# The two row halves of TensorE run opposite products in step, instead of one half trailing the other

## The chip, the cores and the metric

The program runs on one core of a Trainium2 chip. The metric is the time of the kernel on the device in microseconds (us). One profiled execution is shown beside the timed ones: its span runs from the first to the last event on the core. Engines are TensorE (PE, its weight loads PEld), VectorE (DVE), ScalarE (ACT), GpSimd (POOL) and SyncE (SP), which only starts transfers.

## The reference

The input `x` is 2 x 4096 tokens of 192 channels. A causal convolution over 7 tokens comes first, with one softmaxed set of taps for each of 8 heads (24 channels a head). Two feed-forward layers of width 2048 follow:

```python
x = conv(x, softmax(weight))                 # 8192 tokens x 192
h = x @ w_in;   y = max(0.01 * h, h) @ w_out             # "leaky" layer
h = y @ w_in2                                            # "smooth" layer
g = 0 where h <= -1;  h where h >= 1;  (h + 1)**2 / 4 between
out = g @ w_out2
```

All operands are fp32. The kernel splits each operand into a rounded part (hi) and the rest (lo) and adds the products that matter, so that one product becomes several matmuls.

## The kernel before

**Tiles and jobs.** Tokens are worked in 16 tiles of 512. A tile passes two layers, each one is a job: 32 jobs of 16 chunks, a chunk being 128 of the 2048 hidden columns. Job 0 and 1 are leaky jobs of the tiles 0 and 1; then smooth and leaky jobs alternate; jobs 30 and 31 are smooth.

**A chunk.** The first product fills `hidden[c % 4]` (one PSUM bank of four). ACT copies it to `pre` (L767; in a smooth job a Relu, L769, and a Square, L774), DVE makes `g` (L1079 or L1084), ACT rounds it to `g_hi` (`round_g`, L786), DVE subtracts for `g_lo` (L1090). The second product adds the chunk to `acc_edge` and `acc_main`. Two chunks `c`, `c + 1` are always handled together: DVE makes both `g_lo` after the second `g`.

**TensorE in halves.** A contraction of 128 rows is cut into the rows 0 to 63 (`top`) and 64 to 127 (`bottom`), which run as separate 64-row matmuls side by side and add into the same bank one after the other. For two chunks the first product takes 9 matmuls in each half and the second 10 (4 on `acc_edge`, 6 on `acc_main`). `two_chunks(job, c)` writes 19 pairs of one matmul for each half by hand; I call such a place a slot, and one call of `two_chunks` a round. In a round, slots 0 to 8, the top half makes the first product of `c` and `c + 1`, and in slots 9 to 18 the second product of `c - 4` and `c - 3`. The bottom half follows the top: it adds its part of the first product in slots 8 to 16, and its part of the second product in slots 17 and 18 and, in the next round, 0 to 7. Banks pass from half to half by the semaphores `hidden_top_made`, `edge_top_added`, `edge_bottom_added`, `main_top_added` and `main_bottom_added`.

**What holds ACT.** `g_hi` and `g_lo` have four buffers each. ACT may round chunk `c` only once the second product of chunk `c - 4` is complete: `round_g` waits for `main_bottom_added`.

**Work between.** A smooth job's ACT and DVE streams carry the work of other tiles at fixed chunks: the taps of the next tile's convolution (`edge_tap`, chunks 0 to 6), its rounding (`main_hi`, `edge_hi` at chunk 7, `main_lo`, `edge_lo` at chunk 8: L1002, L1054, L1062), and the turn-over of a leaky result into the next operand (`take_edge`, `round_between` on ACT at chunk 9: L803, L808; `between_sum` at chunk 10, `between_main` and `between_edge_hi` at chunk 11 on DVE: L1096, L1102, L1109). Job 0 and 1 also round 16 pieces of weights (ACT L850 to L857, POOL L423 to L433) that SP loads.

**The ends.** The first chunks of job 0 are written in `opening`. After the last round the bottom half finishes its trailing part alone, and the last four chunks' second product runs on the whole array (`whole_edge`, `whole_main`: L611 to L625).

Of the kernel before, what the change touches and what calls it, by code (L numbers as in the profile page):

```python
# [24 lines left out]
P = 128  # L25
T = 512
# [9 lines left out]
JOB_0_MAIN_TAPS = {0: 1, 1: 2, 2: 3, 3: 4, 4: 5, 5: 6}  # L36
JOB_0_EDGE_TAPS = {7: (0,), 8: (1,), 9: (2, 3), 10: (4,), 11: (5, 6)}
PIECE_AT = ({1: 3, 3: 4, 5: 5, 7: 6, 9: 7, 13: 8}, {1: 9, 3: 10, 7: 11, 9: 12, 11: 13, 13: 14, 15: 15})
TAP_LAST = (1, 3)
# [15 lines left out]
def bass_conv_mlp_mlp(nc, x, weight, moe_w_in, moe_w_out, moe2_w_in, moe2_w_out, out):  # L55
# [24 lines left out]
    with ExitStack() as ctx:  # L80
# [106 lines left out]
        hidden_top_made = sem("hidden_top_made")  # L187
        edge_top_added = sem("edge_top_added")
# [83 lines left out]
        last_main = hidden[3][:, 0:T - SPLIT]  # L272
# [40 lines left out]
        def _(sp):  # L313
# [49 lines left out]
            load_w_out(1)  # L363
            load_x_edge(ODD, 0)
            load_w_out(2)
            for piece in range(AHEAD, 2 * PIECES):
                sp.wait_ge(stage_used, piece - AHEAD + 1)
                load_w_in(piece)
# [21 lines left out]
        def _(pool):  # L390
# [52 lines left out]
            low_w_out(2)  # L443
            low_w_out(AHEAD)
            for n in (0, 1):
                for c, piece in PIECE_AT[n].items():
                    if piece > AHEAD:
                        pool.wait_ge(g_lo_ready, CHUNKS * n + c + 1)
                        low_w_in(piece)
                        low_w_out(piece)  # L450
# [10 lines left out]
        def _(pe):  # L461
# [6 lines left out]
            def top_first(job, c, i):  # L468
# [6 lines left out]
                if is_number(n, 0) and c == 0:  # L475
                    if i == 0:
                        pe.wait_ge(main_rounded, 1)
                        pe.wait_ge(first_rounded, 1)
                        pe.wait_ge(w_in_hi, 1)
                    if i == 1:  # L480
                        pe.wait_ge(first_main_ready, 1)
                    if i == 2:
                        pe.wait_ge(weights_ready, 1)
                    if i == 3:
                        pe.wait_ge(edge_hi_ready, 2)
# [25 lines left out]
            def bottom_first(job, c, i):  # L511
# [4 lines left out]
                if i == 0:  # L516
                    pe.wait_ge(hidden_top_made, CHUNKS * n + c + 1)
# [5 lines left out]
                elif i == 3:  # L523
                    last = c % 2 == 0
                    if is_number(n, 0, 1) and c == 0:
                        pe.wait_ge(op1_ready, n + 1)
# [16 lines left out]
            def top_second(job, c, i):  # L543

# [5 lines left out]
                w, hi, lo = w_out[l][top, k], g_hi[k % SLOTS][top, :], g_lo[k % SLOTS][top, :]  # L550
                edge, main = acc_edge[a], acc_main[a]
                if i == 0:
                    if is_number(n, 0, 2):
                        pe.wait_ge(stage_used, l_piece(n, c) + 1)
                    if c == 0 and reached(n, 2):
                        pe.wait_ge(acc_taken, n - 1)
                    if c > 0:
                        pe.wait_ge(edge_bottom_added, (PAIRS - 1) * n + c // 2)
# [3 lines left out]
                elif i in (1, 3):  # L562
                    pe.wait_ge(g_lo_ready, CHUNKS * n + k + 1)
                    done = nc.tensor.matmul(edge[:], w[:, P:2 * P], lo, start=False, stop=False)  # L564
                    if i == 3:
                        done.then_inc(edge_top_added, 1)
                elif i in (4, 7):
                    if i == 4 and c > 0:
                        pe.wait_ge(main_bottom_added, (PAIRS - 1) * n + c // 2)
# [3 lines left out]
                else:  # L573
                    done = nc.tensor.matmul(main[:], w[:, 0:P], lo, start=False, stop=False)  # L574
                    if i == 9:
                        done.then_inc(main_top_added, 1)

            def bottom_second(job, c, i):
# [6 lines left out]
                w, hi, lo = w_out[l][bottom, k], g_hi[k % SLOTS][bottom, :], g_lo[k % SLOTS][bottom, :]  # L585
                edge, main = acc_edge[a], acc_main[a]
                if i in (0, 2):
                    if i == 0:
                        pe.wait_ge(edge_top_added, PAIRS * n + c // 2 + 1)
                    nc.tensor.matmul(edge[:], w[:, P:2 * P], hi, start=False, stop=False)  # L590
                elif i in (1, 3):
                    done = nc.tensor.matmul(edge[:], w[:, P:2 * P], lo, start=False, stop=last and i == 3)  # L592
                    if i == 3:
                        done.then_inc(acc_edge_ready if last else edge_bottom_added, 1)
                elif i in (4, 7):
                    if i == 4:
                        pe.wait_ge(main_top_added, PAIRS * n + c // 2 + 1)
# [3 lines left out]
                else:  # L601
                    done = nc.tensor.matmul(main[:], w[:, 0:P], lo, start=False, stop=last and i == 9)  # L602
                    if i == 9:
                        done.then_inc(acc_main_ready if last else main_bottom_added, 1)
# [24 lines left out]
            def second_half(job, c):  # L629

                for i in range(3):
                    top_second(job, c - 4, i)
                    bottom_first(job, c, i + 1)
                for i in range(5):
                    top_second(job, c - 4, i + 3)
                    bottom_first(job, c + 1, i)
                for i in range(2):
                    top_second(job, c - 4, i + 8)  # L640
                    bottom_second(job, c - 4, i)

            def opening(job):

                for c, i in ((0, 0), (0, 2), (1, 0), (1, 2), (0, 1), (0, 3), (0, 4)):
                    top_first(job, c, i)
                for i in range(2):
                    top_first(job, 1, 2 * i + 1)  # L650
                    bottom_first(job, 0, i)
                for i in range(2):
                    top_first(job, 2, i)
                    bottom_first(job, 0, i + 2)
                for i in range(3):
                    top_first(job, 2, i + 2)
                    bottom_first(job, 1, i)
                for i in range(2):
                    top_first(job, 3, i)
                    bottom_first(job, 1, i + 3)  # L660
                for i in range(2):
                    top_first(job, 3, i + 2)
                    bottom_first(job, 2, i)
                for i in range(2):
                    top_first(job, 4, i)
                    bottom_first(job, 2, i + 2)
                for i in range(3):
                    top_first(job, 4, i + 2)
                    bottom_first(job, 3, i)
                for i in range(2):  # L670
                    top_first(job, 5, i)
                    bottom_first(job, 3, i + 3)
                for i in range(2):
                    top_first(job, 5, i + 2)
                bottom_first(job, 4, 0)
                second_half(job, 4)

            def two_chunks(job, c):

                for i in range(5):
                    top_first(job, c, i)
                    bottom_second(job, c - 6, i + 2)
                for i in range(3):
                    top_first(job, c + 1, i)
                    bottom_second(job, c - 6, i + 7)
                top_first(job, c + 1, 3)
                bottom_first(job, c, 0)
                second_half(job, c)  # L690

            def run(job):
                opens = is_number(job["n"], 0)
                if opens:
                    opening(job)
                for c in range(6 if opens else 0, CHUNKS, 2):
# [50 lines left out]
        def _(act):  # L747
# [13 lines left out]
            def before(job, c):  # L761
# [3 lines left out]
                act.wait_ge(hidden_ready, k + 1)  # L765
# [486 lines left out]
```

## Time and profile before

| | us |
|---|---|
| median of 3 runs (lowest to highest) | 1123.32 (1122.94 to 1123.82) |
| the profiled execution's own time | 1123.96 |
| its span | 1122.2 |
| PE busy in the span | 1117.6 |
| DVE busy | 897.8 |
| ACT busy | 799.1 |
| POOL busy | 53.8 |

Busy times add what overlaps within an engine's pipeline, so an engine at 80% may have fewer free moments than it seems. A row of a timeline has the start, the duration, the engine, the line and the tiles written and read; `x2` merges instructions that follow at once; the bracket says how long the engine stood still before it and what ended that.

### The profile page before, as it was taken

The numbers are of one execution on the slowest core, as the hardware profiler recorded it, in microseconds if no ns is written. First come the engines' busy times: TensorE is split into PE (matmuls) and PEld (weight loads), VectorE is DVE, ScalarE is ACT, GpSimd is POOL, SyncE is SP. The second block draws the span as 40 slices with busy tenths as digits, with TensorE's granted clock in tenths as the row PEclk, the third lists the DMA queues.
The fourth block names the chain that finished last, engine by engine and source line by source line (L and its number), as shares of the span: only waits on it lengthen the run. The fifth ranks groups of instructions, "written<-read, shape, count | busy, mean of one in ns | idle before, by whom it ended". The sixth has DMA issues, their size and how long they took to land.

```text
span 1122.2 us, 25759 instructions
## 1 busy us (share of the span) xinstructions
PE 1117.6 (100%) x9758; PEld 1102.8 (98%) x9758; DVE 897.8 (80%) x1512; ACT 799.1 (71%) x1476; POOL 53.8 (5%) x86
## 2 busy tenths in 40 slices
PE   9999999999999999999999999999999999999998
PEld 8889999999999999999999999999999999999998
DVE  7888877788778887788878888887788877888665
ACT  6878677586775857768577675866758677686786
POOL 7451000000000000000000000000000000000000
PEclk9999999999999999999999999999999999999999
DMA  6330100101001010010100101010010100100001
GB/s 143 103 76 2 27 4 2 30 2 29 2 1 30 1 30 1 3 28 1 29 1 11 21 1 30 1 15 16 1 30 1 26 6 1 30 1 15 1 1 29
DMA packets 112872, 21.95 MB, mean 20 GB/s; under 512 B 104048, under 2 KB 112752, under 8 KB 112752
## 3 DMA queue, kind: packets, MB, share of 16 engines
q1 hardware_dynamic: 110192, 19.81, 9.6%
q8 instruction: 77, 1.26, 0.5%
q10 hardware_dynamic: 2560, 0.52, 0.2%
q14 instruction: 43, 0.35, 0.1%
HBM read 14.02 MB, written 6.29 MB: 18 GB/s over the span
## 4 chain that ended last, share of the span: by engine, by line
PE 100%; DVE 0%; ACT 0%; issue 0%
PE hidden L506 11%; PE hidden L500 7%; PE hidden L504 7%; PE hidden L502 7%; PE acc_main L570 7%; PE acc_main L574 7%; PE acc_main L572 7%; PE acc_edge L564 7%; PE acc_edge L561 7%; PE acc_main L602 3%; PE acc_main L600 3%; PE acc_main L598 3%; PE hidden L520 3%; PE hidden L522 3%; PE hidden L518 3%; PE hidden L527 3%
## 5 line engine op out<-in xcount | busy, mean ns | idle before, releaser
L786 ACT CAST g_hi<-g 128x512 fp32r<-128x512 f32 x510 | 299.5, 618 | 267.2 <-PE acc_main L602 198.5
L1090 DVE TENSOR_TENSOR g_lo<-g,g_hi 128x512 fp32r<-128x512 f32 x510 | 335.1, 690 | 93.9 <-ACT g_hi L786 89.1
L1084 DVE SCALAR_TENSOR_TENSOR g<-hidden,pre 128x512 f32<-128x512 f32 x256 | 176.7, 690 | 101.5 <-ACT pre L774 96.1
L506 PE MATMUL hidden<-op_edge,w_edge 64*128 64x512 f32 x768 | 255.8, 386 | 0.0
L518 PE MATMUL hidden<-op_hi,w_main 64*128 64x512 f32 x512 | 197.9, 387 | 0.0
L500 PE MATMUL hidden<-op_hi,w_main 64*128 64x512 f32 x512 | 197.9, 386 | 0.0
L522 PE MATMUL hidden<-op_hi,w_main 64*128 64x512 f32 x512 | 197.9, 386 | 0.0
L527 PE MATMUL hidden<-op_edge,w_edge 64*128 64x512 f32 x512 | 197.7, 386 | 0.0
L520 PE MATMUL hidden<-op_lo,w_main 64*128 64x512 f32 x512 | 197.7, 386 | 0.0
L502 PE MATMUL hidden<-op_lo,w_main 64*128 64x512 f32 x512 | 197.7, 386 | 0.0
L504 PE MATMUL hidden<-op_hi,w_main 64*128 64x512 f32 x512 | 197.7, 386 | 0.0
L564 PE MATMUL acc_edge<-g_lo,w_out 64*128 64x512 f32 x508 | 196.2, 386 | 0.0
L598 PE MATMUL acc_main<-g_hi,w_out 64*128 64x512 f32 x508 | 196.2, 386 | 0.0
L590 PE MATMUL acc_edge<-g_hi,w_out 64*128 64x512 f32 x508 | 196.2, 386 | 0.0
L592 PE MATMUL acc_edge<-g_lo,w_out 64*128 64x512 f32 x508 | 196.1, 386 | 0.0
L574 PE MATMUL acc_main<-g_lo,w_out 64*128 64x512 f32 x508 | 196.1, 386 | 0.0
L570 PE MATMUL acc_main<-g_hi,w_out 64*128 64x512 f32 x508 | 196.1, 386 | 0.0
L602 PE MATMUL acc_main<-g_lo,w_out 64*128 64x512 f32 x508 | 196.1, 386 | 0.0
L572 PE MATMUL acc_main<-g_hi,w_out 64*128 64x512 f32 x508 | 196.1, 386 | 0.0
L600 PE MATMUL acc_main<-g_hi,w_out 64*128 64x512 f32 x508 | 196.1, 386 | 0.0
L561 PE MATMUL acc_edge<-g_hi,w_out 64*128 64x512 f32 x508 | 196.1, 386 | 0.0
L1079 DVE SCALAR_TENSOR_TENSOR g<-hidden,pre 128x512 f32<-128x512 f32 x256 | 172.6, 680 | 16.5 <-ACT pre L767 13.3
(143 smaller groups left out, 2784.8 us busy)
## 6 DMA issues: line engine op xcount, KB each, us to landing
x_in<-in_x_dram SPq DMA_DIRECT2D x65, 64.0 KB, 2.2
out_dram<-y_main SPq DMA_DIRECT2D x60, 64.0 KB, 1.8
stage<-in_moe_w_out_dram SPq DMA_DIRECT2D x16, 192.0 KB, 2.9
x_in_edge<-in_x_dram SPq DMA_DIRECT2D x66, 32.0 KB, 1.9
stage<-in_moe_w_in_dram SPq DMA_DIRECT2D x32, 64.0 KB, 2.4
out_dram<-y_edge SPq DMA_DIRECT2D x32, 64.0 KB, 1.8
stage<-in_moe_w_in_dram SPq DMA_DIRECT2D x15, 128.0 KB, 2.4
x_in<-in_x_dram ACTq DMA_DIRECT2D x3, 64.0 KB, 3.3
```

What stands on the lines that cost most here:

```text
L500: nc.tensor.matmul(h[:], w_main[l][top, 0, cols], op_hi[l][b][top, :], start=True, stop=False)
L502: nc.tensor.matmul(h[:], w_main[l][top, 0, cols], op_lo[l][b][top, :], start=False, stop=False)
L504: nc.tensor.matmul(h[:], w_main[l][top, 1, cols], op_hi[l][b][top, :], start=False, stop=False)
L506: done = nc.tensor.matmul(h[:], w_edge[l][top, i - 3, cols], op_edge[l][b][top, :], start=False, stop=False)
L518: nc.tensor.matmul(h[:], w_main[l][bottom, 0, cols], op_hi[l][b][bottom, :], start=False, stop=False)
L561: nc.tensor.matmul(edge[:], w[:, P:2 * P], hi, start=k == 0, stop=False)
L564: done = nc.tensor.matmul(edge[:], w[:, P:2 * P], lo, start=False, stop=False)
L570: nc.tensor.matmul(main[:], w[:, 0:P], hi, start=k == 0, stop=False)
L572: nc.tensor.matmul(main[:], w[:, 2 * P:], hi, start=False, stop=False)
L574: done = nc.tensor.matmul(main[:], w[:, 0:P], lo, start=False, stop=False)
L786: nc.scalar.copy(hi_of(n, c)[:], g[c % SLOTS][:]).then_inc(g_hi_ready, 1)
L1090: nc.vector.tensor_tensor(lo_of(n, c)[:], g[c % SLOTS][:], hi_of(n, c)[:].bitcast(F32), ALU.subtract).then_inc(g_lo_ready, 1)
```

## The change

`two_chunks` keeps its 19 slots, but the halves are set against each other: while the top half makes the first product of `c` and `c + 1` (slots 0 to 8), the bottom half starts the second product of `c - 4` and `c - 3` (slots 0 to 9); then the top half completes that second product (slots 9 to 18), and the bottom half completes the first one (slots 10 to 18). No part is left to the next round.

```diff
             def two_chunks(job, c):
                 for i in range(5):
                     top_first(job, c, i)
-                    bottom_second(job, c - 6, i + 2)
-                for i in range(3):
+                    bottom_second(job, c - 4, i)
+                for i in range(4):
                     top_first(job, c + 1, i)
-                    bottom_second(job, c - 6, i + 7)
-                top_first(job, c + 1, 3)
-                bottom_first(job, c, 0)
-                second_half(job, c)
+                    bottom_second(job, c - 4, i + 5)
+                top_second(job, c - 4, 0)
+                bottom_second(job, c - 4, 9)
+                for i in range(4):
+                    top_second(job, c - 4, i + 1)
+                    bottom_first(job, c, i)
+                for i in range(5):
+                    top_second(job, c - 4, i + 5)
+                    bottom_first(job, c + 1, i)
```

The bottom half now opens the second product, so it is the one that waits for `g_hi_ready`, `g_lo_ready` and `acc_taken`; the top half closes it, and ACT's wait names it:

```diff
             def round_g(n, c):
                 if c % 2 == 0 and not ends(n, c):
                     if c >= 4:
-                        act.wait_ge(main_bottom_added, (PAIRS - 1) * n + c // 2 - 1)
+                        act.wait_ge(main_top_added, (PAIRS - 1) * n + c // 2 - 1)
```

`opening` now holds the first six chunks, written out pair by pair (`both((0, 0), (1, 0))`: the top half works on chunk 0 while the bottom half works on chunk 1, then they swap), with waits for `halves_opened` where they swap. ACT then waits for two halves in either order. In job 0 the convolution of tile 1, its rounding and the weights' pieces stand at later or other chunks, with w_in and w_out rounded apart:

```diff
-JOB_0_MAIN_TAPS = {0: 1, 1: 2, 2: 3, 3: 4, 4: 5, 5: 6}
-JOB_0_EDGE_TAPS = {7: (0,), 8: (1,), 9: (2, 3), 10: (4,), 11: (5, 6)}
+JOB_0_MAIN_TAPS = {3: (1, 2), 5: (3, 4), 7: (5, 6)}
+JOB_0_EDGE_TAPS = {9: (0, 1), 10: (2,), 11: (3, 4), 12: (5, 6)}
...
-                    if is_number(n, 0) and c == 11:
+                    if is_number(n, 0) and c == 13:
                         edge_hi(job["finish"])
                         edge_low(job["finish"])
-                    if is_number(n, 0) and c == 13:
+                    if is_number(n, 0) and c == 14:
                         edge_top(job["finish"])
...
-                        if c == 13:
+                        if c == 14:
                             edge_lo(job["finish"])
```

At the end the eight matmuls of the bottom half alone are gone, and the whole-array part runs pair by pair of chunks:

```diff
-            for i in range(2, 10):
-                bottom_second(last_jobs[-1], CHUNKS - 6, i)
-            for c in range(CHUNKS - 4, CHUNKS):
-                whole_edge(JOBS - 1, 1, SMOOTH, c)
-            for c in range(CHUNKS - 4, CHUNKS):
-                whole_main(JOBS - 1, 1, SMOOTH, c)
+            for pair in (CHUNKS - 4, CHUNKS - 2):
+                for c in (pair, pair + 1):
+                    whole_edge(JOBS - 1, 1, SMOOTH, c)
+                for c in (pair, pair + 1):
+                    whole_main(JOBS - 1, 1, SMOOTH, c)
```

TensorE, before, where a round reaches the second product: from the last first-product matmul of the top half (L506, slot 8) to slot 12.

```order
L506 MATMUL hidden<-op_edge,w_edge 128x512
L518 MATMUL hidden<-op_hi,w_main 128x512 [waits hidden_top_made]
L561 MATMUL acc_edge<-g_hi,w_out 128x512 [waits g_hi_ready,edge_bottom_added]
L520 MATMUL hidden<-op_lo,w_main 128x512
L564 MATMUL acc_edge<-g_lo,w_out 128x512 [waits g_lo_ready]
L522 MATMUL hidden<-op_hi,w_main 128x512
L561 MATMUL acc_edge<-g_hi,w_out 128x512 [waits g_hi_ready]
L527 MATMUL hidden<-op_edge,w_edge 128x512
L564 MATMUL acc_edge<-g_lo,w_out 128x512 [waits g_lo_ready]
```

The waits for `g_hi` and `g_lo` stand at slots 9 to 12 of the round. TensorE, changed, slots 0 to 3 of a round, the first product's matmuls of the top half being L495 to L501 and those of the bottom half on the second product L555 and L558:

```order
L495 MATMUL hidden<-op_hi,w_main 128x512 [waits g_ready]
L555 MATMUL acc_edge<-g_hi,w_out 128x512 [waits g_hi_ready,edge_top_added]
L497 MATMUL hidden<-op_lo,w_main 128x512
L558 MATMUL acc_edge<-g_lo,w_out 128x512 [waits g_lo_ready]
L499 MATMUL hidden<-op_hi,w_main 128x512
L555 MATMUL acc_edge<-g_hi,w_out 128x512 [waits g_hi_ready]
L501 MATMUL hidden<-op_edge,w_edge 128x512
L558 MATMUL acc_edge<-g_lo,w_out 128x512 [waits g_lo_ready]
```

The same four waits now stand at the round's first four slots, nine slots ahead of where they stood. ACT, before, late in job 0: the casts of tile 1 (L829 to L844) and the `pre` of chunks 12 to 15 (L767).

```order
L829 CAST op_edge<-conv_edge 64x256 [waits edge_tapped]
L830 CAST op_edge<-conv_edge 64x256
L837 CAST op_top<-op_edge 64x256 [waits edge_hi_ready]
L767 COPY pre<-hidden 128x512 [waits hidden_ready] x2
L786 CAST g_hi<-g 128x512 [waits main_bottom_added,g_ready]
L786 CAST g_hi<-g 128x512 [waits g_ready]
L850 CAST w_main<-stage 128x256 [waits stage_loaded2]
L851 CAST w_edge<-stage 128x256
L857 CAST w_out<-stage 128x2x192 [waits rows_loaded2]
L844 CAST op_top<-op_edge 64x256 [waits edge_hi_ready]
L767 COPY pre<-hidden 128x512 [waits hidden_ready] x2
```

ACT, changed, the same place (casts L899 to L914, `pre` L837, weights L920 to L927), from chunk 13's `g_hi` to chunk 15's `pre`:

```order
L856 CAST g_hi<-g 128x512 [waits g_ready]
L920 CAST w_main<-stage 128x256 [waits stage_loaded2]
L921 CAST w_edge<-stage 128x256
L927 CAST w_out<-stage 128x2x192 [waits rows_loaded1]
L899 CAST op_edge<-conv_edge 64x256 [waits edge_tapped]
L900 CAST op_edge<-conv_edge 64x256
L907 CAST op_top<-op_edge 64x256 [waits edge_hi_ready]
L837 COPY pre<-hidden 128x512 [waits hidden_ready]
L914 CAST op_top<-op_edge 64x256 [waits edge_hi_ready]
L837 COPY pre<-hidden 128x512 [waits hidden_ready]
```

The three casts moved from ahead of chunk 12's `pre` to between the weights and chunk 14's `pre`, and the fourth between the `pre` of 14 and 15.

## Rows read from the trace of the kernel before

**Rows 1.** The page's first part: busy us, share, count.

```profile
PE 1117.6 (100%) x9758; PEld 1102.8 (98%) x9758; DVE 897.8 (80%) x1512; ACT 799.1 (71%) x1476; POOL 53.8 (5%) x86
```

**Rows 2.** Stretches: PE, PEld, DVE, ACT, POOL busy (count), clock, DMA, GB/s.

```profile
80.00:90.00 10.00, 10.00 (x91) 9.03 (x89) 9.74 (x15) 8.14 (x16) 7.48 (x11) 1.00 0.09 15
100.00:1100.00 1000.00, 1000.00 (x8827) 1000.00 (x8824) 801.12 (x1347) 708.65 (x1286) 0.00 (x0) 1.00 0.08 12
```

**Rows 3.** Waits of ACT: for whom, us in total, times, longest.

```profile
ACT g_hi L786 <- PE acc_main L602: 198.5, 165, 1.7
```

**Rows 4.** Timeline of PE in smooth job 6, one round and more.

```profile
235.32 0.39 PE L527 MATMUL hidden<-op_edge,w_edge 64*128 64x512 f32 x1
...
237.08 0.39 PE L500 MATMUL hidden<-op_hi,w_main 64*128 64x512 f32 x1
...
241.39 0.39 PE L500 MATMUL hidden<-op_hi,w_main 64*128 64x512 f32 x1
...
248.41 0.39 PE L564 MATMUL acc_edge<-g_lo,w_out 64*128 64x512 f32 x1
```

**Rows 5.** Timeline of ACT in smooth job 6, chunks 7 to 10.

```profile
232.74 0.58 ACT L769 ACTIVATE pre<-hidden 128x512 f32<-128x512 f32 x1
...
236.44 0.60 ACT L769 ACTIVATE pre<-hidden 128x512 f32<-128x512 f32 x1
...
240.65 0.62 ACT L786 CAST g_hi<-g 128x512 fp32r<-128x512 f32 x1 [0.88 <-DVE g L1084]
241.30 0.58 ACT L803 COPY edge_b<-acc_edge 64x512 f32<-64x512 f32 x1
```

**Rows 6.** Timeline of DVE in smooth job 6, chunks 6 to 11.

```profile
235.88 1.29 DVE L1090 TENSOR_TENSOR g_lo<-g,g_hi 128x512 fp32r<-128x512 f32 x2
...
239.93 0.69 DVE L1084 SCALAR_TENSOR_TENSOR g<-hidden,pre 128x512 f32<-128x512 f32 x1
...
243.69 0.69 DVE L1084 SCALAR_TENSOR_TENSOR g<-hidden,pre 128x512 f32<-128x512 f32 x1 [1.69 <-ACT pre L774]
...
246.42 1.28 DVE L1090 TENSOR_TENSOR g_lo<-g,g_hi 128x512 fp32r<-128x512 f32 x2
```

**Rows 7.** Timeline of DVE, then PE, where PE once waited for `g_lo`.

```profile
27.24 1.24 DVE L1090 TENSOR_TENSOR g_lo<-g,g_hi 128x512 fp32r<-128x512 f32 x2
...
28.54 0.49 PE L564 MATMUL acc_edge<-g_lo,w_out 64*128 64x512 f32 x1
28.55 0.50 PE L518 MATMUL hidden<-op_hi,w_main 64*128 64x512 f32 x1
28.88 0.39 PE L570 MATMUL acc_main<-g_hi,w_out 64*128 64x512 f32 x1
```

**Rows 8.** Timeline of DVE and PE early in job 2.

```profile
82.98 1.55 DVE L1090 TENSOR_TENSOR g_lo<-g,g_hi 128x512 fp32r<-128x512 f32 x2
...
84.76 0.39 PE L564 MATMUL acc_edge<-g_lo,w_out 64*128 64x512 f32 x1
```

**Rows 9.** Timeline of ACT, then DVE, late in job 0.

```profile
40.74 0.41 ACT L837 CAST op_top<-op_edge 64x256 fp32r<-64x256 f32 x1
...
43.11 0.42 DVE L1054 TENSOR_TENSOR op_edge<-conv_edge,op_edge 64x256 fp32r<-64x256 f32 x1
...
45.84 1.29 DVE L1079 SCALAR_TENSOR_TENSOR g<-hidden,pre 128x512 f32<-128x512 f32 x2 [0.55 <-ACT pre L767]
...
50.31 1.29 DVE L1090 TENSOR_TENSOR g_lo<-g,g_hi 128x512 fp32r<-128x512 f32 x2 [0.18 <-ACT g_hi L786]
```

**Rows 10.** Timeline of PE at its two ends, and DVE's last `g_lo`.

```profile
12.34 0.49 PE L500 MATMUL hidden<-op_hi,w_main 64*128 64x512 f32 x1
...
1110.71 0.39 PE L534 MATMUL hidden<-op_top,w_edge 64*128 64x512 f32 x1
...
1113.23 1.46 DVE L1090 TENSOR_TENSOR op_lo<-g,op_hi 128x512 fp32r<-128x512 f32 x2
...
1117.75 0.39 PE L625 MATMUL acc_main<-op_lo,w_out 128*128 128x512 f32 x1
```

More of the change, by code:

```diff
@@ L363, in _ @@
             load_w_out(1)
+            sp.wait_ge(weights_ready, 1)
+            load_w_in(AHEAD)
             load_x_edge(ODD, 0)
@@ L549, in top_second @@
                 k = c + (i // 2 if i < 4 else (i - 4) // 3)
-                w, hi, lo = w_out[l][top, k], g_hi[k % SLOTS][top, :], g_lo[k % SLOTS][top, :]
+                w, hi, lo = w_out[l][bottom, k], g_hi[k % SLOTS][bottom, :], g_lo[k % SLOTS][bottom, :]
                 edge, main = acc_edge[a], acc_main[a]
@@ L584, in bottom_second @@
                 last = c == CHUNKS - 2
-                w, hi, lo = w_out[l][bottom, k], g_hi[k % SLOTS][bottom, :], g_lo[k % SLOTS][bottom, :]
+                w, hi, lo = w_out[l][top, k], g_hi[k % SLOTS][top, :], g_lo[k % SLOTS][top, :]
                 edge, main = acc_edge[a], acc_main[a]
@@ new lines, in first_part @@
+            def first_part(c, i, part):
+                cols = slice(c * P, (c + 1) * P)
+                if i == 0:
+                    w, x_part = w_main[LEAKY][part, 0, cols], op_hi[LEAKY][EVEN]
+                elif i == 1:
+                    w, x_part = w_main[LEAKY][part, 0, cols], op_lo[LEAKY][EVEN]
+                elif i == 2:
+                    w, x_part = w_main[LEAKY][part, 1, cols], op_hi[LEAKY][EVEN]
+                else:
+                    x_part = op_top[LEAKY][EVEN] if part is bottom and i == 4 else op_edge[LEAKY][EVEN]
+                    w = w_edge[LEAKY][part, i - 3, cols]
+                goes_first = part is (top, bottom)[c % 2]
+                return nc.tensor.matmul(hidden[c % SLOTS][:], w, x_part[part, :], start=goes_first and i == 0,
+                                        stop=not goes_first and i == 3)
@@ new lines, in both, with opened, made, edge_part @@
+            def both(t, b):
+                return first_part(*t, top), first_part(*b, bottom)
+            def opened(halves):
+                halves[0].then_inc(halves_opened, 1)
+                halves[1].then_inc(halves_opened, 1)
+            def made(halves):
+                halves[0].then_inc(hidden_ready, 1)
+                halves[1].then_inc(hidden_ready, 1)
+            def edge_part(k, low, part):
+                g_part = (g_lo if low else g_hi)[k]
+                return nc.tensor.matmul(acc_edge[0][:], w_out[LEAKY][part, k, P:2 * P], g_part[part, :],
+                                        start=part is top and k == 0 and not low, stop=False)
@@ L694, in run @@
                 if opens:
-                    opening(job)
-                for c in range(6 if opens else 0, CHUNKS, 2):
+                    opening()
+                for c in range(OPEN if opens else 0, CHUNKS, 2):
                     two_chunks(job, c)
@@ L1155, in run @@
                     if is_number(n, 0):
-                        if c in JOB_0_MAIN_TAPS and c not in TAP_LAST:
-                            main_tap(job["load"], JOB_0_MAIN_TAPS[c])
-                        if c == 5:
+                        if c == 8:
                             turn_x_edge(job["load"])
```

216 lines of the change are left out of this document (125 added, 91 removed).

## The prediction, made before the changed kernel was run

> **What bounds the kernel now.** I read the page's first part, the stretches, the waits, and then the timelines of PE, ACT and DVE over one smooth job. PE works without a break: in the 1000 us from 100 on it issues 8827 half matmuls and never stands still, at a granted clock of 1.00, which is 2.4 GHz [rows 1, 2]. Two round starts of the same kind lie 4.31 us apart (237.08 and 241.39, with 19 slots between), so one slot is 0.2267 us [rows 4]. Alone in the array, in step or one behind the other, the halves keep this pace, so pairing them otherwise saves no slot inside the loop. The top half does 32 x 16 x 9.5 - 20 = 4844 matmuls, 1098.1 us at this pace, out of a span of 1122.2.
>
> ACT looks idle because it waits for PE: 198.5 us of `g_hi` waits for the release of a buffer [rows 3]. That is spare time on ACT, but not in front of PE. The reader should look for the spare between `g_lo` and the matmul that reads it. In smooth job 6 the `g_lo` of chunks 10 and 11 end at 246.42 + 1.28 = 247.70 [rows 6], and the matmul on chunk 11's starts at 248.41 [rows 4]. A matmul that has to wait costs a little more than the wait: where it happened, `g_lo` ended at 28.48, the matmul started at 28.54, the other half stood as well (28.55), and the next followed 0.34 later instead of 0.23 [rows 7]. So a late `g_lo` delays PE's stream to its own end plus 0.06 + 0.11 = 0.17. The spare of chunk 11 is 248.41 - 247.87 = 0.54 us.
>
> **The change, part by part.**
>
> *The loop.* The waits for `g_hi` and `g_lo` move from slots 9 to 12 to slots 0 to 3 of the same round: nine slots, 2.04 us, less time for ACT and DVE. At the other end the first product is complete at slots 13 and 18 instead of 11 and 16. Whether this costs anything is decided at the longest way from a finished `hidden` to a `g_lo`, which in a smooth job runs from chunk 8 to chunk 11, since on it stand the other tiles' steps: Relu of 8 at 236.44 [rows 5], Square, `g` of 8, three roundings of the next tile, `g` of 9 at 239.93 [rows 6], `g_hi` of 9 at 240.65, L803 and L808 at once behind it [rows 5], Relu and Square of 10, `g` of 10 at 243.69, the sum, `g` of 11, two more steps, and both `g_lo` to 247.70 [rows 6]. Each link follows the one before within some 0.03 us (239.93 + 0.69 = 240.62, then 240.65); no wait for PE stands in it. It takes 247.70 - 236.44 = 11.26 us and cannot shrink, as both engines go from one link to the next.
>
> The changed schedule gives it less. From the start of the matmul that completes chunk 8 (slot 13) to the one that reads `g_lo` of chunk 11 (slot 3, three rounds on) are 57 - 10 = 47 slots, 10.65 us. Needed are the matmul itself 0.39, 0.03 to ACT, 11.26, and 0.17 to PE: 11.85. PE stands for 1.20 us. A check from the other side: spare 0.54, less 2.04, plus 0.25 because the Relu of 8 began later (236.44) than `hidden` would allow it even with slot 13 (235.32 + 0.45 + 0.39 + 0.03 = 236.19 [rows 4]), plus the 0.06 by which the bottom half trails: -1.19. Both halves wait, since a matmul behind the waiting one in PE's queue waits as well [rows 7]. This recurs in the 14 smooth jobs that carry both kinds of steps: 14 x 1.20 = 16.8 us. The nearest rows bound one such stall at 0 (the chain hidden as now) and 1.5 (nothing of the late Relu regained); I take 1.20, with 0.9 to 1.4 for the range. Job 30 lacks the next tile's roundings: 0 to 1.2, taken as 0.2. Job 31 and the leaky jobs have no such chain: 0.
>
> *ACT's release.* `round_g` now waits for the top half's end of the second product, slot 18 of the round, where it was slot 7 of the next. It comes 8 slots earlier, but is not in the chain: nothing, hidden behind the `g` of the same pair.
>
> *Jobs 0 and 1.* Early in job 2 DVE is 9.74 of 10 us busy [rows 2]. There the last `g_lo` of job 1 ends at 84.53, and the matmul on it starts at 84.76 [rows 8]: with 0.17 for the way, the spare is 0.06. DVE dictates this matmul now and will then; but it stands nine slots earlier in its round. So all later rounds start 2.04 - 0.06 = 1.98 us later, plus whatever DVE itself is late. What PE lost or won before, in the opening and through job 0, is swallowed by this. DVE's own delay comes late in job 0: three casts of 0.41 to 0.43 move in front of chunk 14's `pre`, which DVE already waits for, and the two subtractions of 0.43 move from ahead of a pair of `g_lo` to between the `g` of 14 and 15 [rows 9]. That is 1.28 + 0.86 = 2.14 at most and 0 at least; DVE stood idle for 0.55 and 0.18 around there [rows 9], which leaves 1.41. I take 1.3. The same number of DVE, ACT and POOL instructions is issued; SP issues as many transfers, with w_in of a piece now ahead of its w_out, and weights arrive while PE still works on the pieces before. I count both as 0, hidden behind DVE's lateness; uncovered they would add what they are late.
>
> *The end.* Before, the last chunk's first product starts its last matmul at 1110.71, slot 16, and the last matmul of all starts at 1117.75 [rows 10], 7.04 later, eight matmuls of the bottom half alone among it (1.81). After, that matmul is at slot 18, 0.45 later. Then 10 whole matmuls on chunks 12 and 13 follow, but those on 14 and 15 wait for DVE: `g_lo` of 15 ends at 1113.23 + 1.46 = 1114.69 [rows 10], 3.98 behind the matmul; with 0.17, and six more matmuls of 0.23, the last starts 5.51 behind it. Gained: 7.04 - 5.51 - 0.45 = 1.08, call it 1.1; bounds 0 and 1.81.
>
> *Sum.* 1.98 + 1.3 + 16.8 + 0.2 - 1.1 = 19.2 us. The profiled execution took 1123.96 for a span of 1122.2; the median of the runs is 0.64 lower, 1123.32. I predict 1123.3 + 19.2 = 1142.5.
>
> **The rivals.**
>
> *More places stall.* In the same job the pair 6 and 7 comes close: Relu of 7 at 232.74 [rows 5], `g_lo` at 235.88 + 1.29 = 237.17 [rows 6]: 4.43, with 0.39, 0.03 and 0.17 it is 5.02 of 23 slots or 5.21 us. Spare 0.19. If ACT or DVE come to it 0.5 us later, since the stream behind a stall is packed more tightly, it adds 0.3 x 14 = 4, and a second such place as much: 1151. Against it: each stall gives both engines 1.2 us to catch up.
>
> *The loop keeps up, only the start is late.* If the chain is 1.2 us shorter on the chip than I read it, 16.8 and 0.2 fall away: 1125.5. For it speaks that ACT is busy for 71% alone [rows 1]; against it that its idle time does not stand in the chain.
>
> *The whole stream of ACT and DVE closes up, and nothing is slower.* It decides from the point at which the chain takes less than 10.65 - 0.59 = 10.06 us and the `g_lo` at 84.53 comes 2 us sooner. For it: brackets of idle time stand before DVE's `g` (1.69 us at 243.69 [rows 6]). But that one waits for Square behind L803, which waits for nothing. Then both halves start at 12.34 [rows 10] and the single matmuls go: 1123.3 - 1.1 = 1122.2.
>
> *The pace changes.* If the halves now took turns without hindering one another, a slot would shrink, for 4864 slots. Nothing in the rows supports another pace: 0.2267 holds over 1000 us, and the whole-array matmuls at the end follow at 0.23 too. The Trainium skill, page "TensorE: Matmul & The Clock Gate", section "Wait — 56ns, not 53.3ns?", gives N / 2.4 GHz plus about 2.5 ns between starts, 215.7 ns for 512 columns. This trace disagrees, with 226.7 ns, and the measurement decides. By that rule in the changed kernel alone, the sum would be 4864 x 0.011 = 53 us lower and each stall 0.5 higher, some 1096.
>
> *The hand-over between halves fails its purpose.* The top half needs the bottom half's part of `acc_main` four slots after it was issued, 0.91 us, against 0.39 + 0.17 = 0.56. Spare 0.35 in each of 256 rounds. Were it missed by 0.1, the time would be 26 us more, 1168. Against it: even a matmul right behind a wait lasts 0.50 [rows 7], which would leave 0.24.
>
> **How the numbers follow.** Forecast 0.80; more places 0.07; only the start 0.05; closed up 0.04; pace 0.01; hand-over 0.03. The forecast's own bounds: 1.98 + 0 + 14 x 0.9 + 0 - 1.8 = 12.8, and 1.98 + 2.1 + 14 x 1.4 + 1.2 - 0.5 = 24.4, with the terms hardly all at one end: 1136 to 1147. To reach part of the first rival the range ends at 1149. A measurement tells 0.2% from no change, 2.2 us. Slower by more: forecast, more places, hand-over and part of "only the start", 0.92. Within: the rest of that and most of "closed up", 0.05. Faster: 0.03.
>
> **What the profile after would show.** PE's waits should list the second product's first `g_lo` of the bottom half on `g_lo` of DVE, some 15 times at about 1 us in smooth jobs, and the round that reads chunks 10 and 11 should be 5.5 instead of 4.3 us long, all others 4.31. From 100 to 1000 the count of PE's matmuls per 100 us falls by 1.7%. Job 2 should begin 3 us later. At the end no run of single bottom matmuls stands, and PE waits once more before the last chunks. I am wrong if no such wait stands in the loop; if the slot is not 0.2267; if the clock leaves 1.00; or if stalls stand in leaky jobs.

## The result, and the profile after

| | before | after |
|---|---|---|
| median of 4 runs (lowest to highest), us | 1123.19 (1122.94 to 1123.82) | 1143.85 (1143.36 to 1144.49) |
| the profiled execution's own time, us | 1123.96 | 1143.36 |
| its span, us | 1122.2 | 1141.6 |

The changed kernel is slower: ratio 1.0183, 95% interval 1.0166 to 1.0201, which is clear of no change. The forecast was 1142.5. The medians lie 20.7 us apart and the two spans 19.4: the profiled execution of before was 0.8 above its median, that of after 0.5 below. The sum of the prediction (19.2) was made on one profile, so the table below holds it against 19.4; most of the 1.3 us between the two differences is explained there (*The opening, and luck*).

The page's first part answers to [rows 1], and the stretches to [rows 2]:

```profile
PE 1124.9 (99%) x9758; PEld 919.7 (81%) x9758; DVE 899.6 (79%) x1512; ACT 816.3 (71%) x1476; POOL 52.4 (5%) x86
```

```profile
80.00:90.00 10.00, 10.00 (x84) 7.32 (x83) 9.73 (x15) 7.96 (x16) 7.57 (x11) 1.00 0.05 7
...
100.00:1100.00 1000.00, 989.14 (x8674) 809.97 (x8674) 790.45 (x1331) 709.69 (x1260) 0.00 (x0) 1.00 0.08 12
```

The clock is 1.00 as before. From 100 to 1100 us PE issues 8674 matmuls in place of 8827, 1.7% fewer, which is the share that was forecast. PE's waits (total, times, longest) now name `g_lo`:

```profile
PE acc_edge L558 <- DVE g_lo L1157: 11.2, 15, 0.8
```

Fifteen waits are 14 smooth jobs and one in job 0, where PE reads chunk 8:

```profile
35.52 0.50 PE L558 MATMUL acc_edge<-g_lo,w_out 64*128 64x512 f32 x1 [0.38 <-DVE g_lo L1157]
```

The 11.2 us are idle time alone. What a round loses is more, and is read from round to round. PE in smooth job 6, where it reads chunks 10 and 11 (L495 opens a round in the top half; L555 and L558 are the bottom half's first matmuls on `g_hi` and `g_lo`):

```profile
250.96 0.39 PE L495 MATMUL hidden<-op_hi,w_main 64*128 64x512 f32 x1
251.18 0.39 PE L555 MATMUL acc_edge<-g_hi,w_out 64*128 64x512 f32 x1
251.19 0.39 PE L497 MATMUL hidden<-op_lo,w_main 64*128 64x512 f32 x1
252.35 0.50 PE L558 MATMUL acc_edge<-g_lo,w_out 64*128 64x512 f32 x1 [0.78 <-DVE g_lo L1157]
252.35 0.50 PE L499 MATMUL hidden<-op_hi,w_main 64*128 64x512 f32 x1
...
252.95 0.50 PE L558 MATMUL acc_edge<-g_lo,w_out 64*128 64x512 f32 x1
252.96 0.50 PE L501 MATMUL hidden<-op_edge,w_edge 64*128 64x512 f32 x1
...
256.49 0.39 PE L495 MATMUL hidden<-op_hi,w_main 64*128 64x512 f32 x1
```

From L495 to L495 it is 256.49 - 250.96 = 5.53 us, against 4.31 in [rows 4]: 1.22 lost, with the top half standing still beside the bottom one (252.35). The same 5.52 to 5.54 stands in 14 rounds, 70.1 us apart, one to each ordinary smooth job. From the third round of job 2 to job 30 all others have 4.31 to 4.33, and the one of job 30 has 4.47. Earlier, the last two rounds of job 0 and the first of job 1, which start at 34.5, 39.7 and 44.4, take 5.13, 4.77 and 4.92, and the last round of job 1 and the first two of job 2 take 4.55, 4.66 and 4.68, where before all of these had 4.31 to 4.34.

ACT and then DVE in the same job, answering to [rows 5, 6]:

```profile
241.63 0.60 ACT L839 ACTIVATE pre<-hidden 128x512 f32<-128x512 f32 x1
...
246.49 0.58 ACT L873 COPY edge_b<-acc_edge 64x512 f32<-64x512 f32 x1
247.10 0.59 ACT L878 CAST op_hi<-acc_main 128x512 fp32r<-128x512 f32 x1
247.58 0.61 ACT L839 ACTIVATE pre<-hidden 128x512 f32<-128x512 f32 x1
```

```profile
242.93 0.69 DVE L1151 SCALAR_TENSOR_TENSOR g<-hidden,pre 128x512 f32<-128x512 f32 x1
243.54 0.68 DVE L1069 TENSOR_TENSOR op_lo<-conv_main,op_hi 128x512 fp32r<-128x512 f32 x1
244.23 0.42 DVE L1121 TENSOR_TENSOR op_edge<-conv_edge,op_edge 64x256 fp32r<-64x256 f32 x1
244.66 0.42 DVE L1129 TENSOR_TENSOR op_edge<-conv_edge,op_top 64x256 fp32r<-64x256 f32 x1
...
250.69 0.67 DVE L1169 TENSOR_TENSOR op_lo<-acc_main,op_hi 128x512 fp32r<-128x512 f32 x1
251.28 0.41 DVE L1176 CAST op_edge<-edge_sum 64x512 fp32r<-64x512 f32 x1
251.62 1.28 DVE L1157 TENSOR_TENSOR g_lo<-g,g_hi 128x512 fp32r<-128x512 f32 x2
```

From the Relu of chunk 8 (241.63) to the end of `g_lo` of chunk 11 (251.62 + 1.28 = 252.90) it is 11.27 us, and 0.05 later L558 starts. Before, it was 11.26 with PE not waiting for it.

Early in job 2, DVE and then PE, answering to [rows 8]:

```profile
84.01 1.55 DVE L1157 TENSOR_TENSOR g_lo<-g,g_hi 128x512 fp32r<-128x512 f32 x2
```

```profile
85.62 0.50 PE L558 MATMUL acc_edge<-g_lo,w_out 64*128 64x512 f32 x1
```

DVE ends at 85.56 in place of 84.53, and the matmul follows 0.06 later. At the end, PE as in [rows 10]:

```profile
1134.16 0.39 PE L605 MATMUL acc_edge<-op_hi,w_out 128*128 128x512 f32 x1
1134.51 0.50 PE L607 MATMUL acc_edge<-op_lo,w_out 128*128 128x512 f32 x1
1134.84 0.40 PE L605 MATMUL acc_edge<-op_hi,w_out 128*128 128x512 f32 x1
1135.29 0.50 PE L607 MATMUL acc_edge<-op_lo,w_out 128*128 128x512 f32 x1
...
1136.75 0.39 PE L619 MATMUL acc_main<-op_lo,w_out 128*128 128x512 f32 x1
```

No run of single bottom matmuls is left, and two short waits for `op_lo` stand in the last pair. L619 at 1136.75 is the last matmul of the second product; as before, four small transposing matmuls on `stage` and `conv_main` follow it. Behind them, ACT's last copy and the last transfer that SP starts, first before, then after:

```profile
1119.14 0.37 ACT L948 COPY stage<-hidden 128x256 f32<-128x256 f32 x1 [0.31 <-PE hidden L742]
1119.54 0.39 SPq L386 DMA_DIRECT2D out_dram<-stage  x1
```

```profile
1138.14 0.37 ACT L1015 COPY stage<-hidden 128x256 f32<-128x256 f32 x1 [0.32 <-PE hidden L809]
1138.85 0.51 SPq L392 DMA_DIRECT2D out_dram<-stage  x1
```

### The profile page after: what moved, and what is told of

Read it like the earlier page. It is cut to its first block, busy times and chain, and to the rows that moved or that the text cites. A ratio compares the mean times of both kernels' runs of the same rounds, so it can differ in the third digit from the quotient of the medians.

```text
span 1141.6 us, 25765 instructions
## 1 busy us (share of the span) xinstructions
PE 1124.9 (99%) x9758; PEld 919.7 (81%) x9758; DVE 899.6 (79%) x1512; ACT 816.3 (71%) x1476; POOL 52.4 (5%) x86
## 4 chain that ended last, share of the span: by engine, by line
PE 79%; DVE 10%; ACT 6%; issue 4%; DVEq 0%; ACTq 0%
PE acc_edge L558 9%; PE acc_main L564 8%; PE acc_main L566 8%; PE acc_main L568 8%; PE hidden L522 8%; PE hidden L517 8%; PE acc_edge L555 8%; PE hidden L513 8%; PE hidden L515 8%; PE hidden L529 4%; DVE g_lo L1157 3%; ACT pre L839 2%; DVE g L1151 2%; ACT pre L844 2%; DVE op_lo L1069 1%
## 5 line engine op out<-in xcount | busy, mean ns | idle before, releaser
L856 ACT CAST g_hi<-g 128x512 fp32r<-128x512 f32 x510 | 315.0, 618 | 107.7 <-DVE g L1151 54.3
L837 ACT COPY pre<-hidden 128x512 f32<-128x512 f32 x256 | 149.6, 587 | 153.0 <-PE hidden L522 92.2
L501 PE MATMUL hidden<-op_edge,w_edge 64*128 64x512 f32 x759 | 255.9, 389 | 0.0
L558 PE MATMUL acc_edge<-g_lo,w_out 64*128 64x512 f32 x506 | 199.7, 395 | 11.2 <-DVE g_lo L1157 11.2
L495 PE MATMUL hidden<-op_hi,w_main 64*128 64x512 f32 x506 | 195.5, 386 | 0.0
L497 PE MATMUL hidden<-op_lo,w_main 64*128 64x512 f32 x506 | 195.4, 386 | 0.0
L555 PE MATMUL acc_edge<-g_hi,w_out 64*128 64x512 f32 x506 | 195.4, 386 | 0.0
```

Source lines behind the costliest of these rows:

```text
L501: done = nc.tensor.matmul(h[:], w_edge[l][top, i - 3, cols], op_edge[l][b][top, :], start=False, stop=False)
L555: nc.tensor.matmul(edge[:], w[:, P:2 * P], hi, start=k == 0, stop=False)
L856: nc.scalar.copy(hi_of(n, c)[:], g[c % SLOTS][:]).then_inc(g_hi_ready, 1)
```

## The experiments

The theory is the prediction's: one chain of ACT and DVE links is longer than the slots between the end of chunk 8 and the matmul on `g_lo` of chunk 11, and each link in it costs its full length in 14 jobs. The rivals are a general lack of pace of ACT and DVE, and the banks' hand-over.

**spread.** Six steps and a cast of the turn-over move to later chunks of the ordinary smooth jobs; each `if c == turn + ...` now reads its own number. The seven numbers of a row are the chunks of `take_edge`, `round_between`, `between_sum`, `between_main`, `between_edge_hi`, `between_edge_lo` and `top_smooth`; job 1 and job 30 keep the old ones:

```diff
+TURNS_1 = (5, 5, 6, 7, 7, 8, 7)
+OLD_TURNS = (9, 9, 10, 11, 11, 12, 11)
+TURNS = (11, 13, 12, 14, 13, 15, 15)
...
-                    turn = 5 if is_number(n, 1) else 9
-                    if job["prev"] and job["prev"][0] == LEAKY and c == turn:
+                    turns = TURNS if not is_number(n, 1, JOBS - 2) else OLD_TURNS if is_number(n, JOBS - 2) else TURNS_1
+                    if job["prev"] and job["prev"][0] == LEAKY and c == turns[0]:
                         take_edge(n - 1, 1 - job["a"])
```

> The changed kernel, with the turn-over of a leaky result (take_edge, round_between, between_sum, between_main, between_edge_hi, between_edge_lo, top_smooth) moved in the 14 ordinary smooth jobs from chunks 9 to 12 to chunks 11 to 15, one or two to a pair. The number of instructions stays the same. Theory (one chain of ACT and DVE links from the Relu of chunk 8 to g_lo of chunk 11 is longer than the 47 slots it has): the two ACT casts and three DVE steps leave that chain, the 14 stalls of 1.22 us go, 17.1 us less, 1126.8 us. Rival (ACT and DVE as a whole can't keep pace with slots 0 to 3, whatever the order): the same work, so the same loss at other chunks, about 1143.9. Rival (the halves disturb one another at the hand-over of banks): 1143.9, too.

Measured: 1127.36 us (1126.75 to 1127.67), ratio to before 1.0035 (1.0022 to 1.0047). The stretch has its count back:

```profile
100.00:1100.00 1000.00, 1000.00 (x8820) 1.00 0.08 12
```

The 5.53 rounds are gone; eight of 4.36 or 4.37 are left, each the round that reads chunks 14 and 15 of a smooth job, where the turn-over now ends. DVE's work is the same (897.3 us busy, 899.6 in the changed kernel), so it is not the amount of work that held PE but which steps stood between two chunks. Both rivals fall.

**hi_first.** The order of the bottom half's second product:

```diff
             def bottom_second(job, c, i):
 
+                i = (0, 2, 4, 5, 1, 3, 7, 8, 6, 9)[i]
```

> The changed kernel, with the bottom half's ten matmuls of the second product in another order: both on g_hi for acc_edge, two on g_hi for acc_main, then both on g_lo for acc_edge (slots 4 and 5 in place of 1 and 3), then the rest. Theory (the stall is a late g_lo of chunks 10 and 11): g_lo of chunk 11 is wanted two slots, 0.45 us, later and that of chunk 10 three slots later; each of 14 stalls shrinks from 1.22 to 0.7 or 0.8, 6 to 7 us less in all, 1137 to 1138 us. Rival (it is g_hi or the bank's hand-over that holds the round): nothing changes, 1143.9.

Measured: 1136.54 us (1136.48 to 1136.68), 7.3 less than the changed kernel and a little past the 6 to 7 expected. The 14 rounds take 5.07 to 5.13, 0.76 to 0.82 too long in place of 1.22: the two slots, 0.45, come back nearly in full, 6.1 us in all, and another 0.6 stands up to job 2 and in job 30. `g_hi` of chunk 11 is read a slot earlier in this run and the bank `acc_main` two slots earlier, and still the stall shrinks: it is `g_lo` that is waited for.

**dose_after** and **dose_before2.** The same subtraction made again, once in the changed kernel and twice in the kernel before (`DOSE` stands for the 1 or 2 of the two runs):

```diff
                 dve.wait_ge(op2_hi_ready, t + 1)
+                if reached(n, 2) and not is_number(n, JOBS - 2):
+                    for i in range(DOSE):
+                        nc.vector.tensor_tensor(op_lo[SMOOTH][b][:], acc_main[a][:],
+                                                op_hi[SMOOTH][b][:].bitcast(F32), ALU.subtract).then_inc(again, 1)
+                        dve.wait_ge(again, DOSE * (t - 1) + i + 1)
```

> The changed kernel, with the subtraction of between_main made twice in each of the 14 ordinary smooth jobs (chunk 11), the second after the first has ended: 0.7 us more on DVE inside the chain. Theory (chain without spare): all of it comes out at PE, 14 x 0.7 = 10 us more, 1153 to 1154 us. Rival (DVE is idle for a fifth of the time and takes it up, the stall has another cause): 1143.9.

> The kernel before, with the subtraction of between_main made three times in each of the 14 ordinary smooth jobs (chunk 11), each after the end of the one before: 2 x 0.7 = 1.4 us more on DVE inside the same chain. Theory (the chain is there too, with 0.54 us of spare before the matmul on g_lo of chunk 11): 1.4 - 0.54 = 0.86, or a little more for the second wait that a stall brings, 14 times: 12 us more, 1135 us. Rival (with the halves one behind the other such a delay is taken up, as the spare is larger than read): 1123.3.

Measured: 1154.50 us (1154.12 to 1154.63), 10.65 more than the changed kernel; and 1136.10 us (1135.91 to 1137.16), 12.75 more than before. By rounds, the 14 of dose_after take 6.23 to 6.27 in place of 5.53, 0.73 for each dose; in dose_before2 the first two take 5.61 and 5.25 and the other twelve 5.18 to 5.21 in place of 4.31, 0.88 for two doses. PE's waits, first of dose_after, then of dose_before2:

```profile
PE acc_edge L559 <- DVE g_lo L1158: 21.4, 15, 1.5
```

```profile
PE acc_edge L565 <- DVE g_lo L1091: 6.5, 14, 0.9
```

In the changed kernel the dose comes out at PE whole, though DVE is idle for a fifth of the time. In the kernel before, 2 x 0.73 = 1.46 come out as 0.88, so 0.58 were free: the spare read as 0.54 from [rows 4, 6] was there.

**taps_later.** spread and hi_first together, and three of job 1's main taps in job 2 (its DVE loop begins one pass later, with job 2 written out):

```diff
-                        if 0 <= c - job["taps_at"] < TAPS:
+                        if 0 <= c - job["taps_at"] < TAPS - (LATE_TAPS if is_number(n, 1) else 0):
...
+                        if is_number(n, 2):
+                            if c in (8, 9, 10):
+                                main_tap(job["finish"] + (1,), TAPS - LATE_TAPS + (8, 9, 10).index(c))
```

> spread and hi_first in one kernel, and on top of them the last three of the seven main taps of tile 2 (about 0.8 to 1.3 us of DVE each) moved from job 1 to chunks 8 to 10 of job 2, its rounding to chunks 11 to 13. Theory (at the end of job 1 and in the first rounds of job 2 DVE dictates the time, 0.97 us of the delay stand there): that delay goes, job 2's rounds stay at 4.31, the small rests of 0.06 in the loop go too: 1125.2 us. Rival (the 0.97 are those of another wait): as spread less 0.7 for the order of the matmuls, 1126.7.

Measured: 1126.11 us (1125.30 to 1126.35), ratio to before 1.0021 (1.0011 to 1.0030), between the two expectations. The stretch that was in question is clear. From 70 to 95 us, first in spread, then in taps_later:

```profile
70.00:95.00 25.00, 24.95 (x216) 1.00 0.23 52
```

```profile
70.00:95.00 25.00, 25.00 (x224) 1.00 0.23 51
```

The long rounds at the end of job 1 and in job 2 (4.50, 4.66 and 4.72 in spread) are 4.31. In their place the last round of job 2 and the first of job 3, where what the moved taps and their roundings delay comes due, take 4.56 and 4.51: 0.45 of the 0.97 were given back.

**combined.** taps_later and job 0 spread anew:

```diff
-JOB_0_MAIN_TAPS = {3: (1, 2), 5: (3, 4), 7: (5, 6)}
-JOB_0_EDGE_TAPS = {9: (0, 1), 10: (2,), 11: (3, 4), 12: (5, 6)}
+JOB_0_MAIN_TAPS = {1: (1,), 3: (2, 3), 5: (4, 5), 7: (6,)}
+JOB_0_EDGE_TAPS = {8: (0,), 9: (1, 2), 10: (3,), 11: (4, 5), 12: (6,)}
...
-                        if c == 10:
+                        if c == 9:
                             main_lo(job["finish"])
```

The turn of the edge tile (`turn_x_edge` on DVE, `move_half` on ACT) moves from chunk 8 to 7 as well.

> taps_later, with job 0's work spread anew: main taps one pair earlier (chunks 1, 3, 5, 7), the turn of the edge tile at chunk 7 in place of 8, edge taps from chunk 8, main_lo at chunk 9, casts where the changed kernel has them. Theory (1.8 us are lost between chunk 10 of job 0 and chunk 4 of job 1 because DVE comes to g_lo and to the operands of tile 1 too late): most of it goes, 1.9 us less than taps_later, 1123.3 us, as the kernel before. By its shorter end (1.1 us) it can be no faster than 1122.3. Rival (the 1.8 us belong to the weights' arrival or the new opening): 1125.2.

Measured: 1123.86 us (1123.44 to 1124.90) in 11 runs beside 1123.54 of before, ratio 1.0004 (0.9995 to 1.0013): no difference that can be told. Its stretches of 30 to 60 and on:

```profile
30.00:60.00 30.00, 30.00 (x267) 1.00 0.46 118
...
100.00:1100.00 1000.00, 1000.00 (x8823) 1.00 0.08 12
```

Against 251 matmuls from 30 to 60 in taps_later. So what PE lost behind the opening of job 0 was due to the order of the other work on DVE (and one step of ACT), as the places of the weights and the code of `opening` are the same in both. Twenty of the 20.7 us are back with the paired halves kept; the gain of the shorter end does not show in the time. In its profile the last matmul of the second product starts 0.9 earlier than in before's, and the span is 0.5 shorter, but that profile has the early one of two openings (told of below) and before's the late one, 0.8 us apart.

**tail_by_kind.** spread, with the old order of the whole-array part:

```diff
-            for pair in (CHUNKS - 4, CHUNKS - 2):
-                for c in (pair, pair + 1):
-                    whole_edge(JOBS - 1, 1, SMOOTH, c)
-                for c in (pair, pair + 1):
-                    whole_main(JOBS - 1, 1, SMOOTH, c)
+            for c in range(CHUNKS - 4, CHUNKS):
+                whole_edge(JOBS - 1, 1, SMOOTH, c)
+            for c in range(CHUNKS - 4, CHUNKS):
+                whole_main(JOBS - 1, 1, SMOOTH, c)
```

> spread, with the whole-array part at the end in the order of the kernel before: first all four chunks on acc_edge, then all four on acc_main. Theory (the mains of chunks 12 and 13 hide the wait for g_lo of 14 and 15): 1.4 us more than spread, 1128.7 us, and the two waits at the end grow from 0.3 to 1.3 us together or more. Rival (the gain of the new end is the eight single matmuls only): 1127.4.

Measured: 1128.01 us (1127.58 to 1128.73), 0.65 more than spread, with intervals that overlap (1.0040, 1.0024 to 1.0055): the time alone does not settle it. The trace does:

```profile
1117.74 0.51 PE L608 MATMUL acc_edge<-op_hi,w_out 128*128 128x512 f32 x1 [0.75 <-ACT op_hi L858]
1118.55 0.50 PE L610 MATMUL acc_edge<-op_lo,w_out 128*128 128x512 f32 x1 [0.31 <-DVE op_lo L1160]
```

The mains of chunks 12 and 13 no longer cover the wait. The two waits are 1.1 us together, under the 1.3 or more expected. From the start of the last round to the last matmul of the second product it is 1.4 us longer than in spread, as expected. The span is only 0.9 longer: the last round starts 0.2 earlier in this profile, and from that last matmul to the end it is 4.5 us in place of 4.9, as the edge result leaves 2.0 us ahead of SP's last transfer in place of 0.9.

**edge_last.** spread, with the order of the bottom half changed so that its bank is ready just in time:

```diff
+                i = (0, 2, 4, 5, 7, 8, 1, 3, 6, 9)[i]
```

> spread, with the bottom half's acc_edge matmuls on g_lo at slots 6 and 7, just ahead of the top half's slot 9, which needs that bank: two slots between in place of six. This measures the price of a hand-over that comes too late. Theory (a matmul's 0.39, 0.06 to PE and 0.11 behind a wait, 0.56 in all, against 0.45): 0.1 us in each of some 250 rounds, 1150 us. If the bottom half stays one start behind the top one, as it does in the changed kernel, it is 0.33 a round, 1210 us. Rival (a bank needs no such time): 1127.4.

Measured: 1167.94 us, one run. From 54 us on, all rounds take 4.48. One of them, around slot 9 (L562 is the bottom half on `g_lo`, L588 the top half on the same bank):

```profile
602.26 0.39 PE L562 MATMUL acc_edge<-g_lo,w_out 64*128 64x512 f32 x1
602.49 0.39 PE L504 MATMUL hidden<-op_edge,w_edge 64*128 64x512 f32 x1
602.49 0.39 PE L572 MATMUL acc_main<-g_lo,w_out 64*128 64x512 f32 x1
602.71 0.50 PE L588 MATMUL acc_edge<-g_hi,w_out 64*128 64x512 f32 x1
602.72 0.50 PE L572 MATMUL acc_main<-g_lo,w_out 64*128 64x512 f32 x1
603.05 0.40 PE L590 MATMUL acc_edge<-g_lo,w_out 64*128 64x512 f32 x1
```

L588 starts exactly on time (602.26 + 0.45), takes 0.50, and its successor follows after 0.34. So a hand-over at two slots costs 0.11 at once and 0.17 in the round; I had expected 0.10 or 0.33, and neither case was right on the size. The mechanism of the prediction's rival on the hand-over is real, but in the changed kernel it never fires: its closest hand-over, of `acc_main`, has three slots, 0.68 us (the prediction read four), and its rounds take 4.31.

## Why the prediction was right, point by point

| step | predicted, us | in the trace, us |
|---|---|---|
| 14 smooth jobs | 14 x 1.20 = 16.8 | 14 x 1.22 = 17.1 |
| job 30 | 0.2 | 0.16 |
| all up to the third round of job 2 | 1.98 + 1.3 = 3.3 | 2.8 |
| the end | -1.1 | -1.1 at the last matmul of the second product, 0.4 of it lost behind it |
| sum | 19.2 | 19.4 |

*The loop.* The chain kept its length to 0.01 us, and the matmul that completes chunk 8 starts at 241.21 and the Relu at 241.63, so 0.39 and 0.03 held. Three experiments show the chain from three sides: a link out (spread), two slots more (hi_first), a link in (both doses). No second place stalls in the ordinary smooth jobs, which was the first rival.

*Up to job 2.* At job 2 DVE dictates the matmul, as forecast, and comes 1.03 later, not 1.3. The wait moved by eight slots, not nine, as two rows of each trace show. First before, in a round whose slot 0 is 237.08 [rows 4] (slot 11 of both halves), then after (slot 1 of the top half, slot 0 of the bottom half):

```profile
239.57 0.39 PE L561 MATMUL acc_edge<-g_hi,w_out 64*128 64x512 f32 x1
239.63 0.39 PE L527 MATMUL hidden<-op_edge,w_edge 64*128 64x512 f32 x1
```

```profile
106.63 0.39 PE L555 MATMUL acc_edge<-g_hi,w_out 64*128 64x512 f32 x1
106.63 0.39 PE L497 MATMUL hidden<-op_lo,w_main 64*128 64x512 f32 x1
```

The bottom half trailed by 0.06 before and is a whole slot behind now. So 8 x 0.2267 = 1.81 took the place of 2.04. In the loop this does not count, as both ends of the chain lie in the bottom half.

Three statements of this step were wrong, though its sum came out near. First, DVE's lateness did not swallow what PE had lost before. Of the 2.8 us, 1.8 stood already at chunk 4 of job 1 and 1.0 came at the end of job 1 and in the first rounds of job 2. In chunks 4 to 11 of job 1 each `g_lo` comes 1.0 later than before, while DVE is busy for only 4.1 of each 5 us from 60 to 70: DVE follows PE there and keeps the lateness. In spread, with the same code up to job 2 and an opening 0.8 later, DVE ends the first `g_lo` of job 2 1.85 later than before, against 1.06 in the changed kernel.

Second, the place. The forecast had three casts and two subtractions make DVE late at the `g_lo` of chunks 14 and 15 of job 0. Those do come 1.29 and 1.21 later, but the round that reads them loses only 0.06. PE lost 1.2 in the two rounds before, waiting for `g_lo` of chunks 8 to 11 (the 35.52 above is the first), and 0.6 in the first round of job 1, waiting for tile 1's operand itself: at 45.43 for the second of the moved casts (it ends at 45.38) and at 48.09 for the second of the moved subtractions (it ends at 48.03).

Third, job 2 began 2.1 us late, not 3. And by the letter one sign of being wrong came true: stalls stand in the leaky jobs 0 and 1, though in no leaky job of the loop.

Combined takes back the 1.6 us that PE lost between its first round behind `opening` and chunk 4 of job 1, and half of the 1.0 at job 2. So most of this was the order of the other tiles' work, mainly DVE's.

*The opening, and luck.* The ten profiles show two openings some 0.8 us apart. ACT's first cast of tile 0 (`op_hi`) starts at 9.3 to 9.5 in before, spread, taps_later, tail_by_kind and dose_after, and at 8.5 to 8.8 in the changed kernel, hi_first, combined, edge_last and dose_before2. Before and dose_before2 have the same code there, as have the changed kernel and dose_after, so it is not the kernel that decides; what does is open. Before's profile has the late opening and that of the changed kernel the early one, so 19.4 is about 0.8 too small. With the late opening on both sides (spread or dose_after beside before) the loss up to the third round of job 2 is 3.7 or 3.8, and 1.0 of it stands already at the first round behind the new `opening`: this the forecast had put at nothing. In all it would be about 20.2, beside the 20.7 of the medians. That the table agrees within 0.2 is luck; the forecast was 1.0 to 1.5 short: 0.4 up to job 2, 0.3 in the loop and 0.4 behind the last matmul can be named.

*The end.* The matmuls gained what was worked out. Not seen was that the edge result now leaves 0.9 us before SP's last transfer, where it left 2.0 us before it: from the last matmul of the second product to the end it is 4.9 us in place of 4.5. Most of this shows in the rows above. Before, SP starts that transfer 0.03 after the end of ACT's copy (1119.51); after, it does so 0.33 behind it (1138.52), as it is still issuing the edge result until 1138.80. In tail_by_kind, where the edge result leaves 2.0 us ahead, it is 4.5 again. The last transfers also take longer to land, SP's 2.4 us in place of 1.9; that they hinder one another is argued only.

*The rivals.* The pace stayed at 0.2267 in each kernel, at clock 1.00 (rounds of 4.31 outside the stalls; edge_last, whose hand-over comes late in every round, is the exception). The start alone, without the loop, is what spread shows: 1127.36, where 1125.5 had been worked out. The opening explains part of this: with the same code, the first full round stands 0.2 late in the changed kernel's profile and 1.0 late in that of spread. The rest is in the eight small stalls (0.5), job 30 (0.2) and the end (0.4).

## What to carry to other kernels

When a change makes a consumer read earlier, look for the longest run of links on the producing engines that stand shoulder to shoulder, and hold it against the time between its two fixed ends; the engines' busy share says nothing of it, as 80% and 71% here went with 17 us of waiting. The cure was not less work but another order: the other tiles' steps, placed one or two to a pair of chunks, fit under the same matmuls. A simpler schedule for the bound engine was paid for in slack here, and as it removed no matmul from the loop it could at best break even there, as combined did.

## What was not expected of the hardware

A semaphore that arrives just when the matmul was due does not delay its start, but still costs 0.17 us a round (edge_last: 4.48 against 4.31, the next start after 0.34 in place of 0.23). With three slots in place of two, 0.23 us more, the hand-over of `acc_main` in the changed kernel costs nothing; what lies between was not measured.

The two halves have two positions to one another in the loop, and keep them for hundreds of rounds. In the kernel before their starts are 0.06 apart and in combined 0.08 to 0.14; in the changed kernel and in spread both start within 0.01 us. The page of the profile shows it in the weight loads: busy for 97 or 98% of the span before, in taps_later and in combined, and 77 to 82% in the others, where two loads start together as the matmuls do. The doses do not decide it: dose_before2 has 81%, and its halves start within 0.01 us from 90 to 105 us, before its first dose, where before, with the same code so far, has 0.06. In the traces of before and combined the distance changes where a matmul waits or nearly does: before from 84.76 on, the matmul with next to no spare [rows 8], combined at 112.0 to 112.6, where its second long round begins. What sets the distance there was not tested.

```profile
PE 1123.1 (99%) x9758; PEld 920.6 (81%) x9758; DVE 915.9 (81%) x1540; ACT 801.9 (71%) x1476; POOL 53.9 (5%) x86
```

The slot is the same 0.2267 in both positions, so PEld's share is no measure of TensorE's load here.
